# Gelu's table loaded behind the last exponential, and a turn's first product with x waiting for the low part at its third term

## The reference

```python
kv_pool = kv.reshape(B, H // 4, 4, W // 4, 4, C).mean(axis=(2, 4))
k = v = kv_pool.reshape(B, -1, C) @ w_sr          # 768 keys
a = softmax((q @ k.T) / sqrt(C));  x = a @ v
h = x @ w_in1;  x = (h * sigmoid(1.702 * h)) @ w_out1     # 128 -> 2048 -> 128
h = x @ w_in2;  out = (h * clip(h + 3, 0, 6) / 6) @ w_out2
```

## Time and profile before

| what | value |
|---|---|
| runs of the kernel | 1282.58, 1283.05, 1283.74 us, median 1283.05 |
| profiled execution, first to last instruction (its span) | 1280.9 us |
| TensorE busy | 1271.9 us, 99% |
| VectorE busy | 1037.1 us, 81% |
| ScalarE busy | 1033.3 us, 81% |
| granted TensorE clock, mean | 1.000 |

### The profile page before, as it was taken

The page is one execution under the profiler, slowest core; times in us unless marked ns, Lnnn a source line. Parts: engine busy times, 40 slices in busy tenths (PEclk is TensorE's granted clock), DMA queues, the critical chain, the costliest instruction groups (busy, mean ns, idle before and its releaser), DMA issues.

```text
span 1280.9 us, 18370 instructions
## 1 busy us (share of the span) xinstructions
PE 1271.9 (99%) x5800; PEld 1065.7 (83%) x5800; DVE 1037.1 (81%) x1084; ACT 1033.3 (81%) x1216; POOL 34.4 (3%) x46
## 2 busy tenths in 40 slices
PE   8999999999999999999999999999999999999998
PEld 7888888888888888888888888888888888888887
DVE  5788888888878888888888888887888888887768
ACT  3888878888788888888888878888888888887776
POOL 1800000000000000000000000000000000000000
PEclk9999999999999999999999999999999999999999
DMA  8421321303203123032130220312303213022001
GB/s 282 123 45 38 75 46 28 74 10 64 58 16 74 30 43 74 0 74 49 25 74 14 60 62 12 74 34 40 74 0 74 49 25 74 18 48 66 2 9 17
DMA packets 183685, 65.69 MB, mean 51 GB/s; under 512 B 104560, under 2 KB 176368, under 8 KB 183408
## 3 DMA queue, kind: packets, MB, share of 16 engines
q1 hardware_dynamic: 182576, 65.30, 22.6%
q10 hardware_dynamic: 1088, 0.13, 0.1%
HBM read 22.87 MB, written 6.34 MB: 23 GB/s over the span
## 4 chain that ended last, share of the span: by engine, by line
PE 98%; DMA 1%; DVE 0%; ACT 0%; SPq 0%; issue 0%; DVEq 0%
PE pair L1064 16%; PE pair L1068 16%; PE pair L1065 16%; PE bank_av L1068 9%; PE bank_av L1065 9%; PE bank_av L1064 9%; PE bank_out L1065 7%; PE bank_out L1068 7%; PE bank_out L1064 7%; DMA kv_sb<-in_kv_dram 1%; PE pair L1077 0%; SPq L337 0%; PE bank_av L1077 0%; PE pair L1095 0%; ACT work L520 0%; DVE kv_sb L752 0%
## 5 line engine op out<-in xcount | busy, mean ns | idle before, releaser
L892 DVE TENSOR_TENSOR mid_lo<-work,mid_hi 128x1024 fp32r<-128x1024 f32 (+1 forms) x193 | 234.8, 1217 | 129.2 <-ACT mid_hi L607 129.1
L1064 PE MATMUL pair<-x_hi,w_hi 128*128 128x512 f32 (+1 forms) x774 | 300.6, 388 | 0.0
L1065 PE MATMUL pair<-x_hi,w_lo 128*128 128x512 f32 (+1 forms) x774 | 300.0, 388 | 0.0
L1068 PE MATMUL pair<-x_lo,w_hi 128*128 128x512 f32 (+1 forms) x774 | 299.9, 388 | 0.0
L568 ACT ACTIVATE work<-pair 128x1024 f32<-128x1024 f32 x184 | 189.4, 1030 | 116.5 <-PE pair L1068 114.2
L871 DVE TENSOR_TENSOR mid_lo<-work,mid_hi 128x1024 fp32r<-128x1024 f32 x184 | 223.3, 1213 | 25.1 <-ACT mid_hi L583 25.0
L884 DVE SCALAR_TENSOR_TENSOR work<-work,pair 128x1024 f32<-128x1024 f32 (+1 forms) x194 | 231.6, 1194 | 3.1 <-ACT work L595 2.3
L595 ACT ACTIVATE work<-pair,half 128x1024 f32<-128x1024 f32 (+1 forms) x194 | 212.4, 1096 | 4.7 <-PE pair L1068 4.7
L607 ACT ACTIVATE mid_hi<-work 128x1024 fp32r<-128x1024 f32 (+1 forms) x193 | 201.3, 1043 | 2.3 <-DVE work L884 2.3
L583 ACT ACTIVATE mid_hi<-work 128x1024 fp32r<-128x1024 f32 x184 | 194.3, 1056 | 2.3
L1064 PEld LDWEIGHTS pair<-x_hi,w_hi 128*128 128x128 f32 x774 | 145.3, 188 | 34.9 <-ACT work L568 4.2
(11 more groups left out here) (166 smaller groups left out, 1550.2 us busy)
## 6 DMA issues: line engine op xcount, KB each, us to landing
p_keys<-p_turned SPq DMA_DIRECT2D x368, 96.0 KB, 2.2
inv_b<-inv_dram SPq DMA_DIRECT2D x23, 256.0 KB, 3.3
out_dram<-y_sb SPq DMA_DIRECT2D x92, 64.0 KB, 2.4
q_raw<-in_q_dram SPq DMA_DIRECT2D x88, 64.0 KB, 2.0
kv_sb<-in_kv_dram SPq DMA_DIRECT2D x6, 768.0 KB, 9.4
w_raw<-in_moe_w_in_dram SPq DMA_DIRECT2D x2, 1024.0 KB, 7.9
kv_sb<-in_kv_dram SPq DMA_DIRECT2D x6, 256.0 KB, 8.2
inv_dram<-inv_t SPq DMA_DIRECT2D x92, 0.5 KB
```

The costliest lines, as they stand in the source:

```text
L892: dve.tensor_tensor(in_pair(mid_lo[mid2(t, p)], t, p, c), in_pair(act2[p % 2], t, p, c), in_pair(mid_hi[mid2(t, p)], t, p, c), ALU.subtrac ...
L1064: pe.matmul(dst, a_hi, b_hi, start=start, stop=False)
L1065: pe.matmul(dst, a_lo, b_hi, start=False, stop=False)
L1068: return pe.matmul(dst, a_hi, b_lo, start=False, stop=stop)
```

## The change

On ScalarE, in each turn that has exponentials, `load_table(ACT.Gelu_apprx_sigmoid)` goes from behind `x1_high(i + 1)` to ahead of it. On TensorE, `hidden1` of pair 0 waits for x1's high part ahead of its first matmul, and for x1's low part ahead of its third.

```diff
                     for s in range(1, SLOTS):
                         exponential(i + 2, s)
+                if scored:
+                    load_table(ACT.Gelu_apprx_sigmoid)
                 if with_p:
                     x1_high(i + 1)
-                if scored:
-                    load_table(ACT.Gelu_apprx_sigmoid)
...
             def hidden1(t, p):
-                if p == 0 and later(t):
-                    pe.wait_ge(x1_ready, t + 1)
+                by_terms = p == 0 and later(t)
+                if by_terms:
+                    pe.wait_ge(x1_hi_ready, t + 1)
...
-                hidden(hidden1_in(t, p), 0, p, x1_hi, x1_lo).then_inc(h1_ready, 1)
+                hidden(hidden1_in(t, p), 0, p, x1_hi, x1_lo,
+                       low=(x1_ready, t + 1) if by_terms else None).then_inc(h1_ready, 1)
```

## The result

The changed kernel takes 1289.02 us in the median of five runs (1288.08 to 1289.59), and the kernel before, run beside it, 1283.0 (1282.57 to 1283.74). The ratio is 1.0047, with an interval of 1.0037 to 1.0058: it is slower by 6.0 us. The forecast was 1289.7, with a range of 1286.3 to 1292.3.

A forecast was written before the change was run, and what follows sets the result against it. TensorE was taken to bound the kernel, busy 1271.9 of 1280.9 us. Losses of 0.20 and 0.14, less 0.02 lost before, gave 0.32 us a turn; 21 turns made 6.7, so 1283.05 + 6.7 = 1289.7, range 1286.3 to 1292.3.

The forecast's parts named there:

- VectorE's queue without room: VectorE, from `x1_low` to `act1_lo` 0: no idle time, so everything behind `x1_low` comes 0.51 us late.
- Two waits: TensorE: `project1` 0's third term waits for `act1_lo` 0, then `hidden1` 2 for `gelu` 1; together 0.32 us a turn.
- the second: `hidden1` 2's load behind `gelu` 1, delayed through `act2_hi` 0's wait for `hard_swish` 0: 0.26 us late, loss 0.14.
- The first product with x1: TensorE's `hidden1` 0: first load on time with 0.14 us to spare, third term's load 0.05 late, both free.
- the rule of 0.12: TensorE weight loads: about 0.12 us of lateness is free, and a loss is the lateness less 0.12.
- The ceiling of the gain: TensorE's waits on `gelu`: 0.02 us a turn, 23 times, 0.5 us in all, the most the change could win.
- the covered shift: Rival: `act2_hi` 0 doesn't wait for VectorE, so the time stays at 1282.5 to 1283.5; chance 0.07.
- half of the shift: Rival: `x1_high` on ScalarE shifts only 0.25 to 0.35 us, not 0.51; +1.5 to +3.3 us; chance 0.09.
- the adding up: Rival: waits at the first product's third term, `project1` 0 and `hidden1` 2 cost 0.51 us a turn, 1293.8; chance 0.06.
- The drain: Rival: a 1.38 us pause on ScalarE behind the exponential; 1.7 us a turn, 36 us, 1319; chance 0.01.

The follow-up runs named there:

- filler, 128 columns: Kernel before, plus an unread maximum over 128 columns of x on VectorE behind `x1_low` in the 21 turns: 1283.14 us, ratio 1.0003.
- rounding on GpSimd: Whole change, with x1's high part rounded by GpSimd and not ScalarE in the 21 turns: 1284.84 us, ratio 1.0016.
- filler, 384 columns: Kernel before, plus an unread maximum over 384 columns of x on VectorE behind `x1_low` in the 21 turns: 1288.01 us, ratio 1.0041.
- the gap filled: Whole change, with the transpose of the first probabilities put ahead of `x1_low` on VectorE: 1283.25 us, ratio 1.0004.
- the table load alone: Kernel before with only the table load moved; `hidden1` 0 still waits for both parts of x1 at its first term: 1292.64 us, ratio 1.0075.
- the two swapped kernels: Whole change, on VectorE either with `hard_swish` 0 ahead of the third transpose (1286.88 us) or with `act1_lo` 0 ahead of the fourth (1289.40 us).

## Why the prediction was right

The mechanism held in each step, and the sizes are close; the sum came out 0.7 us high. The delay of VectorE and the cost of it, from the runs:

| kernel | delay of VectorE's queue, us | cost in the median, us | for a turn | a turn's growth in the trace |
|---|---|---|---|---|
| filler, 128 columns | 0.19 | 0.4 (not told from 0) | 0.02 | 0.07 (longest of 11 executions) |
| rounding on GpSimd | 0.30 | 2.1 | 0.10 | 0.10 |
| filler, 384 columns | 0.46 | 5.2 | 0.25 | 0.26 |
| the change | 0.50 | 6.0 | 0.29 | 0.29 |

- *VectorE's queue without room is late by 0.51.* It was 0.50. `x1_high` itself took 0.61 in place of 0.63 us. Nearly the same delay (0.46) without any edit on ScalarE costs nearly the same (5.2 us); with the gap filled the change costs nothing that the medians can tell. This is shown in both directions.
- *Only the part above the slack costs.* Between 0.30 and 0.50 us of delay a turn loses 0.19 for 0.20. By the medians the cost starts near 0.2; the one trace at 0.19 would put it lower, and that is open.
- *Two waits, the later one sets the sum.* Shown by taking each away: without the earlier one 6.65 us stay, without the later one 4.1 us, and with both 6.0. So their prices don't add. The 6.65 and the 6.0 are the same within the intervals, and the turns of the two traces are 52.24 and 52.22 us.
- *The sizes.* I had 0.20 and 0.14 us, less the 0.02 that was lost before, and so 0.32; the rows give 0.18 and 0.08 with some hundredths beside them, and the turn grew by 0.29. The term that was too large is the second. `act2_hi` 0 was late by 0.30 and not 0.32, and `gelu` 1 ended 9.30 us behind `scale_x` for 9.03, 0.27 later and not 0.32. So the load of `hidden1` 2 came 0.20 behind its due time, where I had 0.26. With the first border at 0.26 that is 6.0 us and not 6.7.
- *The first product with x1 costs nothing.* Its loads were 0.05 us late at most. Without the wait by terms I had the first load 0.58 late, which by the rule of 0.12 is 0.46 us a turn; it was 0.57 late, and the median rose by 9.8 us, 0.47 a turn.
- *`gate`.* I had it start 0.2 us sooner; against `scale_x` it is 0.14, as it starts 0.12 and not 0.04 us behind the drawn end of `hidden2`'s last matmul (647.68 + 0.39 to 648.19). This costs nothing, since `gelu` 0 waits for TensorE in any case.
- *The ceiling of the gain.* I had put the 0.02 us a turn lost on `gelu` as what the earlier table load could win. It can't even win this: with VectorE back in step and ScalarE idle ahead of `gate` the row "4.2, 23, 0.2" stood unchanged in the run with the transpose first, and the table load alone left it too. That wait begins with `hidden1` 1's last matmul, which in the kernel before is drawn to 649.60, and `gelu` 1 starts at 649.63, and not with the ScalarE queue.

```profile
649.21 0.39 PE L1068 MATMUL pair<-x_lo,w_hi 128*128 128x512 f32 x1
```

In the changed kernel, where TensorE was done in time, `gelu` 1 starts 1.00 us behind `gate` 1; in the one before and with the transpose first it is 1.02 and 1.03. This reading is argued from the rows; no run moved `hidden1` 1.

Of the rivals, the covered shift fell with `act2_hi` 0, which does wait for `hard_swish` 0, half of the shift with `x1_high` at 1.42 us behind the end of the accumulator's read, the adding up with the turn of 0.29 us more and with the two swapped kernels. The drain that the Trainium skill gives on the page "ScalarE: Activation LUTs", section "What ACT_TABLE_LOAD costs", fell too: the load behind the last exponential starts 0.02 us after the accumulator's read and what follows `warm` starts 0.11 after `warm`'s start; the table's 1283 ns is there, a pause of 1380 ns isn't, in front or behind. The prediction left open what stands in front of a load directly behind an accumulator's read. The trace of the kernel before had one such place, near its start, and could have settled it:

```profile
41.96 0.19 ACT L520 ACTIVATION_READ_ACCUMULATOR probs<-both_banks,neg_max 128x1 f32 x1
42.17 1.28 ACT L617 ACT_TABLE_LOAD   x1
```

No kernel beat the one before. The version with the transpose first matches it within the interval of the medians, with a trace that has turns 0.04 us longer.

## What to carry to other kernels

Where one engine bounds the kernel and hardly waits, look at a moved instruction's followers on the other engines and not only at the engine it runs on: find the queue that has no idle time behind the hand-over, and count the slack to each of its readers. By the medians of these runs a delay cost only what exceeded the smallest of these slacks, and of two waits in a row the later one set the price. When the idle time ahead of an instruction is shorter than what is put into it (0.91 us for 1.42 here), the rest is handed on in full unless some independent work can be pulled forward into the new gap.

## What was not expected of the hardware

GpSimd took 0.35 us from the end of a VectorE instruction to the start of its own, behind two waits in a loop, where ScalarE took 0.04 for the same hand-over; back to VectorE it took 0.03 (643.39 + 0.62 to 644.04). How much of it is the second wait or the loop was not tried. The kernel with 128 columns of filler had turns of 52.00 us from the fourth on and of 51.93 in the two before, and no load at a turn's border that was late by more than 0.14, which the kernel before has too. The median of its runs doesn't show it, and it stays open.
